# Down projections of a gated expert block: seven quarter-block products in place of eight half-block ones, and where the weights for them are prepared

## The chip, the cores and the metric

The kernel runs on one core of a Trainium2 chip (trn2). Its engines run side by side, each through its own list of instructions: TensorE (PE, with the weight loads shown apart as PEld), VectorE (DVE), ScalarE (ACT), GpSimd (POOL) and SyncE (SP), which here only issues transfers. They meet at semaphores. The metric is the device time of one launch in microseconds (us), lower is better; the time of the kernel before is the median of 3 runs.

## What is computed

Cut to what matters:

```
x = local attention with memory keys      # 3072 tokens x 512, kept on chip in Y
x = (x @ w_a * (x @ w_b)) @ w_out         # first block, hidden width 1536
P = exp(x @ w_gate - max); 8 Sinkhorn rounds over tokens and 8 experts
out = 0
for e in range(8):                        # second block
    h = maximum(x @ w1[e], 0)             # w1[e] is 512 x 1024
    out += P[:, e:e+1] * (h @ w2[e])      # w2[e] is 1024 x 512
```

Everything is float32. Products on TensorE are made of three passes over operands that are split into a high part, rounded to fp32r, and a low part that is the rest: high by high, high by low, low by high (`PARTS`).

## The kernel before

The 3072 tokens are three pairs of 1024 (two blocks of 512 each). The second block walks pair by pair, and in a pair through 32 units (`V2`): a unit is a quarter of an expert, 256 of its 1024 hidden columns. So there are 96 units (`M2`), numbered u = 0 to 95 here; pair 0 is u = 0 to 31. A unit has two halves of work on TensorE:

- The up projection, x by the w1 slice, as a 2x2 by 2x2 block product by Winograd's scheme with seven products (`PRODUCTS`, `product`, 6 matmuls of 512 columns each, 42 in all). ScalarE and VectorE join the products in PSUM (`seed`, `copy_u`, `copy_v`, `sum_22`, `sum_21`).
- The down projection, hidden by the w2 slice, as eight plain products (`down`, one for each 128 tokens, 6 matmuls of 512 columns, 48 in all). VectorE adds each to the output in SBUF, times the gate (`accumulate`). ScalarE makes the rectified hidden block's high parts (`h_hi`) and VectorE its low parts (`h_lo`).

On TensorE's list the two are woven together: up product 0 of unit u, down product 0 of unit u-1, up product 1, down product 1, and so on, then an eighth down product.

The weights need preparing once: in pair 0 (`fresh`) each slice is loaded raw from HBM, its operands for the seven products are made (sums on GpSimd in `up_sums`, high parts on ScalarE in `up_hi` and `down_hi`, low parts on GpSimd in `up_lo` and `down_lo`), and the finished form is also written to HBM (`w1_kept`, 1792 KB a unit; `w2_kept`, 1024 KB a unit). Pairs 1 and 2 only fetch it (`fetch_up`, `fetch_down`). The raw loads have two slots, one for w1 and one for w2 in the second block.

The order in pair 0 is written out by hand. On SP, for each u: load the raw w1 slice of u, keep w2 of u-1, load the raw w2 slice of u, keep w1 of u. All transfers sit in this one list, and a wait in it holds all that stand behind it. On GpSimd, for each u: `up_sums` of u+1, `down_lo` of u, `up_lo` of u+1. On ScalarE, for each u: `seed`, `down_hi` of u, first half of `up_hi` of u+1, `copy_u` (the fifth up product of u waits for it), second half of `up_hi`, then the hidden block's parts between `copy_v` and the end. TensorE's first product of unit u+1 waits for all of `up_lo` of u+1 (semaphore `w1_lo`).

Of the kernel before, what the change touches and what calls it, by code (L numbers as in the profile page):

```python
# [12 lines left out]
P = 128  # L13
# [26 lines left out]

def build(nc, q, k, v, mem_k, mem_v, w_a, w_b, w_out, w_gate, w1, w2, out):
    B, H, S, HD = q.shape
# [16 lines left out]
    HP = H // 2  # L59
# [23 lines left out]
    with ExitStack() as ctx:  # L83
# [49 lines left out]
        w2_kept = nc.dram_tensor("w2_kept", [V1 + V2, P, 4 * D], F32).ap()  # L135
# [3 lines left out]
        b_down = bank[3:6]  # L139
        b_lg, b_gate = bank[6], bank[7]  # L140
# [42 lines left out]

        x_sum = sem("x_sum")
# [18 lines left out]
        y_acc = sem("y_acc")  # L203
        s_wg = sem("s_wg")
# [59 lines left out]
        def kept_w2(w):  # L264
            return w % V1 if w < M1 else V1 + (w - M1) % V2
# [74 lines left out]
        def _(sp):  # L340
# [43 lines left out]
            def raw_free(item):  # L384
# [135 lines left out]
        def _(pool):  # L520
# [46 lines left out]
            def clear(r):  # L567
# [5 lines left out]
                else:  # L573
# [3 lines left out]
                                        pattern=[[0, H], [0, none.shape[2]]],  # L577
# [37 lines left out]
            for p in range(1, PAIRS):  # L615
                for i in range(len(X_POOL)):
                    operand_lo(3 + p, p, i)

        @block.tensor
        def _(pe):  # L620
# [145 lines left out]
            def down(w, g):  # L766
# [689 lines left out]
```

## Time and profile before

| | |
|---|---|
| median of 3 runs | 2724.42 us (2721.48 to 2724.61) |
| the profiled execution's own time | 2725.75 us |
| its span, first to last instruction | 2723.8 us |
| TensorE busy | 2660.6 us, 98% |
| TensorE granted clock, mean | 0.991 of full speed |
| VectorE, ScalarE, GpSimd busy | 51%, 28%, 19% |
| mean traffic to and from HBM | 161 GB/s |

The profile is of one execution. "Busy" of an engine is the union of its instructions' times. A matmul's time in the rows runs from its start to the arrival of its last result, so matmuls in a row overlap; what one of them costs is the distance between two starts. The granted clock 1.00 is the level of 2.4 GHz and 0.50 that of 1.2 GHz.

### The profile page before, as it was taken

How to read it: one execution, taken by the hardware profiler on the slowest of the kernel's cores; microseconds unless marked ns; L12 is line 12 of the kernel's file. 1: busy time of each engine (PE TensorE's matmuls, PEld its weight loads, DVE VectorE, ACT ScalarE, POOL GpSimd, SP SyncE). 2: the span in 40 equal slices, each digit the busy share in tenths (PEclk: the TensorE clock that was granted, in tenths of full speed). 3: DMA queues.
4: the chain of work that ended last, by engine and by line, in shares of the span. 5: the costliest groups of instructions: out<-in, count | busy, mean ns of one | idle time of the engine just before them, and what ended most of it. 6: DMA issues, size and time to landing. Idle time of an engine off the chain costs nothing.

```text
span 2723.8 us, 36964 instructions
## 1 busy us (share of the span) xinstructions
PE 2660.6 (98%) x15264; PEld 2194.9 (81%) x15264; DVE 1390.1 (51%) x2039; ACT 774.5 (28%) x1349; POOL 516.9 (19%) x440
## 2 busy tenths in 40 slices
PE   7879999999999999999999999999999999999999
PEld 6768878878777888888888888888888888888887
DVE  3454454544567545545565544544546445445444
ACT  4544432222333333333332222212223212212221
POOL 0055510110444454454430000000001000000000
PEclk9989999999999999999999999999999999999999
DMA  7655643443365555556544343343343443343342
GB/s 182 157 153 207 230 178 139 161 159 140 114 208 174 188 184 207 189 185 209 185 178 159 130 168 128 130 167 128 131 166 128 164 164 128 135 163 128 138 160 89
DMA packets 145542, 437.96 MB, mean 161 GB/s; under 512 B 53216, under 2 KB 101088, under 8 KB 113888
## 3 DMA queue, kind: packets, MB, share of 16 engines
q1 hardware_dynamic: 145376, 435.61, 44.5%
q8 instruction: 121, 1.98, 0.3%
q14 instruction: 45, 0.37, 0.0%
HBM read 308.69 MB, written 126.94 MB: 160 GB/s over the span
## 4 chain that ended last, share of the span: by engine, by line
PE 92%; DVE 4%; issue 1%; ACT 1%; DMA 1%; POOL 1%; SPq 1%; DVEq 0%; ACTq 0%
PE bank L719 44%; PE bank L794 44%; PE bank L642 2%; PE bank L681 1%; DVE tmp L1229 1%; PE bank L657 1%; PE bank L669 0%; DMA Qr<-in_q_dram 0%; DVE Y L1320 0%; DVE Y L1262 0%; PE bank L691 0%; SPq L371 0%; POOL X L563 0%; DVE hid L1325 0%; DVE hid L1381 0%
## 5 line engine op out<-in xcount | busy, mean ns | idle before, releaser
L719 PE MATMUL bank<-X,W 128*128 128x512 f32 x5550 | 1399.8, 391 | 14.7 <-ACT tmp L1032 4.8
L719 PEld LDWEIGHTS bank<-X,W 128*128 128x128 f32 x5550 | 1042.0, 188 | 241.0 <-issue 20.5
L794 PE MATMUL bank<-W,hid 128*128 128x512 f32 x4608 | 1154.2, 389 | 2.8 <-DVE Y L1259 2.8
L794 PEld LDWEIGHTS bank<-W,hid 128*128 128x128 f32 x4608 | 864.8, 188 | 182.9 <-DVE Y L1259 3.2
L1259 DVE SCALAR_TENSOR_TENSOR Y<-bank,gate,Y 128x512 f32<-128x512 f32 x720 | 539.4, 750 | 568.6 <-PE bank L794 561.0
L563 POOL TENSOR_TENSOR X<-Y,X 128x1024 fp32r<-128x1024 f32 x30 | 77.9, 2601 | 1022.6 <-ACT X L984 1022.6
L1090 ACT ACTIVATE hid<-tmp 128x512 fp32r<-128x512 f32 x192 | 121.3, 632 | 354.3 <-DVE tmp L1226 274.2
L794 PE MATMUL bank<-hid,W 128*128 128x512 f32 x864 | 219.3, 389 | 1.2 <-issue 1.2
L1028 ACT ACTIVATE tmp<-bank 128x512 f32<-128x512 f32 x132 | 79.0, 599 | 486.9 <-PE bank L719 486.9
L1381 DVE SCALAR_TENSOR_TENSOR hid<-bank,hid 128x512 fp32r<-128x512 f32 x192 | 132.7, 691 | 162.5 <-ACT hid L1090 162.4
L794 PEld LDWEIGHTS bank<-hid,W 128*128 128x128 f32 x864 | 162.4, 188 | 35.5 <-issue 1.6
L1090 ACT ACTIVATE hid<-bank 128x512 fp32r<-128x512 f32 x192 | 114.9, 598 | 230.6 <-PE bank L719 230.6
L1262 DVE TENSOR_TENSOR Y<-Y,bank 128x512 f32<-128x512 f32 x144 | 98.2, 684 | 153.9 <-PE bank L794 153.5
L1221 DVE TENSOR_TENSOR tmp<-bank,tmp 128x512 f32<-128x512 f32 x132 | 91.3, 692 | 165.3 <-ACT tmp L1032 165.1
L1017 ACT ACTIVATE bank<-bank 128x512 f32<-128x512 f32 x131 | 76.2, 582 | 316.5 <-PE bank L719 316.5
L1032 ACT ACTIVATE tmp<-bank 128x512 f32<-128x512 f32 x132 | 78.9, 597 | 261.4 <-PE bank L719 261.4
L1381 DVE SCALAR_TENSOR_TENSOR hid<-tmp,hid 128x512 fp32r<-128x512 f32 x192 | 145.5, 758 | 6.4 <-ACT hid L1090 0.7
L1226 DVE TENSOR_TENSOR tmp<-bank,tmp 128x512 f32<-128x512 f32 x132 | 91.2, 691 | 70.5 <-PE bank L719 69.6
L552 POOL TENSOR_TENSOR W<-Ws,W 128x512 fp32r<-128x512 f32 x88 | 114.3, 1322 | 23.3 <-ACT W L956 23.3
L557 POOL TENSOR_TENSOR W<-raw,W 128x1024 fp32r<-128x1024 f32 x38 | 91.3, 2402 | 68.0 <-ACT W L965 67.9
L552 POOL TENSOR_TENSOR W<-raw,W 128x512 fp32r<-128x512 f32 x88 | 88.7, 1030 | 42.8 <-ACT W L956 42.8
L541 POOL TENSOR_TENSOR Ws<-raw 128x256 f32<-128x256 f32 x44 | 33.9, 770 | 253.7 <-DMA raw<-in_moe_w_dram 251.7
(87 smaller groups left out, 1066.7 us busy)
## 6 DMA issues: line engine op xcount, KB each, us to landing
W<-w_kept SPq DMA_DIRECT2D x88, 1792.0 KB, 8.6
w_kept<-W SPq DMA_DIRECT2D x44, 1792.0 KB, 6.7
W<-w_kept SPq DMA_DIRECT2D x76, 1024.0 KB, 4.8
w_kept<-W SPq DMA_DIRECT2D x38, 1024.0 KB, 4.9
raw<-in_moe_w_dram SPq DMA_DIRECT2D x64, 512.0 KB, 6.4
Vw<-in_v_dram SPq DMA_DIRECT2D x176, 56.0 KB
Kr<-in_k_dram SPq DMA_DIRECT2D x12, 512.0 KB, 4.8
Qr<-in_q_dram SPq DMA_DIRECT2D x12, 512.0 KB, 4.5
```

Of the source, the lines that this page charges most:

```text
L552: nc.gpsimd.tensor_tensor(w_piece(c, n, 1), w_piece_of(slot, n), w_piece(c, n, 0).bitcast(F32), ALU.subtract).then_inc(w1_lo, 1)
L557: nc.gpsimd.tensor_tensor(W2[:, w % 2, 1, :], raw[:, item_w2(w) % 2, :], W2[:, w % 2, 0, :].bitcast(F32), ALU.subtract).then_inc(w2_lo, 1)
L719: last = nc.tensor.matmul(into[:, :], W1[:, c % 2, ws, w_slot, kc, :], X[:, pos, xs, kc, :], start=(start and kc == 0 and n == 0), stop=(k ...
L794: last = nc.tensor.matmul(into[:, :], lhsT, rhs, start=(j == 0 and n == 0), stop=(j == 1 and n == 2))
L1028: nc.scalar.activation(into, bank[BANK_B][:, :], ACT.Copy).then_inc(c_u, 1)
L1032: nc.scalar.activation(into, bank[BANK_B][:, :], ACT.Copy).then_inc(c_v, 1)
L1090: nc.scalar.activation(hid[:, u % 2, f, l, 0], of, ACT.Relu).then_inc(e_hi, 1)
L1221: nc.vector.tensor_tensor(into, bank[BANK_E][:, :], of, ALU.add).then_inc(c_22, 1)
L1226: nc.vector.tensor_tensor(into, bank[BANK_E][:, :], of, ALU.add).then_inc(c_21, 1)
L1259: nc.vector.scalar_tensor_tensor(out=y, in0=ps, scalar=by, in1=y, op0=ALU.mult, op1=ALU.add).then_inc(y_acc, 1)
L1262: nc.vector.tensor_tensor(y, y, ps, ALU.add).then_inc(y_acc, 1)
L1381: nc.vector.scalar_tensor_tensor(out=hid[:, u % 2, f, l, 1], in0=of, scalar=0.0, in1=hid[:, u % 2, f, l, 0].bitcast(F32), op0=ALU.max, op1 ...
```

## The change

Pair 0's down projections stay as they are. In pairs 1 and 2 (64 units) the down projection becomes a 2x2 by 2x2 block product with seven products as well: the hidden block is cut in halves of tokens and of hidden columns, w2's slice in halves of hidden columns and of output columns. Each of the seven (`down_product`, order and banks in `DOWN`) is 12 matmuls of 256 columns. The products are summed where they land, in PSUM, in two pairs of banks; ScalarE copies the shared first product from one pair to the other (`copy_halves`), and VectorE adds quarter blocks to the output straight from PSUM, 24 additions of 256 columns a unit (`add_blocks`). The seven left operands (`H`) are made in every unit: rectified blocks on ScalarE, four sums (`hidden_sum`) and seven low parts (`hidden_lo`) on GpSimd, seven high parts (`hidden_hi`) on ScalarE. VectorE's `h_lo` goes away there.

The right operands are made in pair 0, beside what was done: GpSimd makes four sums of w2's quarter blocks (`block_sums`) between `up_sums` and `down_lo`, ScalarE their high parts into the raw slot (`t_hi`, placed behind the sixth up product's hidden part), GpSimd their low parts (`block_sums_lo`) as the last step of the unit. Two more transfers a unit keep them (`keep_t_hi`, `keep_t_lo`, 512 KB each), and the raw w2 slot comes free only when both have been made and the first is kept. Pairs 1 and 2 fetch 1792 KB in place of 1024 KB for the down side (`fetch_blocks`). Buffers are laid out anew.

```diff
+DOWN = ((0, 0, 1), (1, 5, 1), (2, 3, 1), (4, 1, 0), (5, 2, 1), (6, 4, 0), (3, 6, 0))
...
+                    if item_w2(w) == item - 2 and w >= M1:
+                        sp.wait_ge(t_lo, w - M1 + 1)
+                        sp.wait_ge(s_th, 16 * (w - M1 + 1))
...
+            def keep_t_hi(u):
+                sp.wait_ge(t_hi, u + 1)
+                sp.dma_start(w2n_kept[u, :, 0, 4:8], b_blocks(M1 + u)).then_inc(s_th, 16)
+
+            def keep_t_lo(u):
+                sp.wait_ge(t_lo, u + 1)
+                sp.dma_start(w2n_kept[u, :, 1, 4:8], T_SUMS).then_inc(s_tl, 16)
...
             for u in range(1, V2):
                 load_up(C1 + u)
                 keep_down(M1 + u - 1)
+                keep_t_hi(u - 1)
                 load_down(M1 + u)
+                keep_t_lo(u - 1)
                 keep_up(C1 + u)
...
+            def block_sums(u):
...
+                nc.gpsimd.tensor_tensor(t1, b12, b11, ALU.subtract).then_inc(t_sum, 1)
+                nc.gpsimd.tensor_tensor(t3, b22, b12, ALU.subtract).then_inc(t_sum, 1)
+                pool.wait_ge(t_sum, 4 * u + 1)
+                nc.gpsimd.tensor_tensor(t2, b22, t1, ALU.subtract).then_inc(t_sum, 1)
+                pool.wait_ge(t_sum, 4 * u + 3)
+                nc.gpsimd.tensor_tensor(t4, b21, t2, ALU.subtract).then_inc(t_sum, 1)
+
+            def block_sums_lo(u):
+                pool.wait_ge(t_hi, u + 1)
+                nc.gpsimd.tensor_tensor(T_SUMS.bitcast(F32R), T_SUMS, b_blocks(M1 + u), ALU.subtract).then_inc(t_lo, 1)
...
             for u in range(V2):
                 if u + 1 < V2:
                     up_sums(C1 + u + 1)
+                block_sums(u)
                 down_lo(M1 + u)
                 if u + 1 < V2:
                     up_lo(C1 + u + 1)
...
+                block_sums_lo(u)
...
+            def down_product(u, q):
...
+                for half in range(2):
...
+                    ps = b_half[pair][half]
+                    for m in range(2):
+                        at = (2 * half + m) * P
+                        for n, (a, b) in enumerate(PARTS):
+                            last = nc.tensor.matmul(ps[:, m * D // 2:(m + 1) * D // 2], H[:, h, a, at:at + P],
+                                                    W2n[k % 2][:, b, blk, :],
+                                                    start=(q in (0, 5) and m == 0 and n == 0),
+                                                    stop=(m == 1 and n == 2), skip_group_check=True)
+                    last.then_inc(p_half, 1)
...
+                act.wait_ge(t_sum, 4 * u + 4)
+                act.wait_ge(w2_lo, kept_w2(w) + 1)
+                nc.scalar.activation(b_blocks(w).bitcast(F32R), T_SUMS, ACT.Copy).then_inc(t_hi, 1)
```

How the lists stand, at the places that the prediction speaks of. First SP's list in pair 0, one unit of it, before; `raw` with four by 256 is the w1 slice, with two by 512 the w2 slice, and `w_kept` is what is kept in HBM:

```order
L413 DMA w_kept<-W 128x3584 [waits w1_lo]
L403 DMA raw<-in_moe_w_dram 128x4x256 [waits w1_lo]
L418 DMA w_kept<-W 128x2048 [waits w2_lo]
L409 DMA raw<-in_moe_w_dram 128x2x512 [waits w2_lo]
L413 DMA w_kept<-W 128x3584 [waits w1_lo]
```

The same stretch of SP's list in the changed kernel, where `w2n_kept` takes the blocks for the seven products:

```order
L465 DMA w_kept<-W 128x3584 [waits w1_lo]
L455 DMA raw<-in_moe_w_dram 128x4x256 [waits w1_lo]
L474 DMA w2n_kept<-W_0 256x1x1024 [waits w2_lo]
L479 DMA w2n_kept<-raw 128x1024 [waits t_hi]
L461 DMA raw<-in_moe_w_dram 128x2x512 [waits s_th,t_lo,w2_lo]
L483 DMA w2n_kept<-tmp 128x1024 [waits t_lo]
L465 DMA w_kept<-W 128x3584 [waits w1_lo]
```

The raw load of w2, and with it all that stands behind it, now waits for `t_lo`; before, it waited for `w2_lo` alone.

GpSimd's list for one unit of pair 0 before (`Ws` holds w1's sums, `W` and `W2` are the split weights):

```order
L541 TENSOR_TENSOR Ws<-raw 128x256 [waits w1_lo,w1_hi,s_raw0]
L542 TENSOR_TENSOR Ws<-raw 128x256
L544 TENSOR_TENSOR Ws<-Ws,raw 128x256 [waits w_sum]
L546 TENSOR_TENSOR Ws<-raw,Ws 128x256 [waits w_sum]
L557 TENSOR_TENSOR W<-raw,W 128x1024 [waits w2_hi]
L552 TENSOR_TENSOR W<-raw,W 128x512 [waits w1_hi]
L552 TENSOR_TENSOR W<-raw,W 128x256 [waits w1_hi]
L552 TENSOR_TENSOR W<-Ws,W 128x512 [waits w1_hi] x2
```

And in the changed kernel, from behind `up_sums` (four rows as above, now lines 631 to 636) to the end of the unit:

```order
L664 TENSOR_TENSOR tmp<-raw 128x256 [waits s_tl,s_raw1]
L665 TENSOR_TENSOR tmp<-raw 128x256
L667 TENSOR_TENSOR tmp<-raw,tmp 128x256 [waits t_sum]
L669 TENSOR_TENSOR tmp<-raw,tmp 128x256 [waits t_sum]
L651 TENSOR_TENSOR W_1<-raw,W_1 128x1024 [waits w2_hi]
L642 TENSOR_TENSOR W<-raw,W 128x512 [waits w1_hi]
L642 TENSOR_TENSOR W<-raw,W 128x256 [waits w1_hi]
L642 TENSOR_TENSOR W<-Ws,W 128x512 [waits w1_hi] x2
L674 TENSOR_TENSOR tmp<-tmp,raw 128x1024 [waits t_hi]
```

Four instructions of 256 columns came in ahead of `down_lo`, and one of 1024 behind `up_lo`.

## Rows read from the trace of the kernel before

**Rows 1.** The page: busy times, and the chain that ended last by engine.
```profile
PE 2660.6 (98%) x15264; PEld 2194.9 (81%) x15264; DVE 1390.1 (51%) x2039; ACT 774.5 (28%) x1349; POOL 516.9 (19%) x440
...
PE 92%; DVE 4%; issue 1%; ACT 1%; DMA 1%; POOL 1%; SPq 1%; DVEq 0%; ACTq 0%
```

**Rows 2.** Windows in pair 0 and pair 2: engines' busy us, clock, DMA share, GB/s.
```profile
1200.00:1400.00 200.00, 200.00 (x883) 165.40 (x882) 103.32 (x140) 70.62 (x118) 96.10 (x81) 1.00 0.54 189
...
2200.00:2600.00 400.00, 400.00 (x1766) 331.21 (x1765) 196.05 (x274) 83.45 (x138) 0.00 (x0) 1.00 0.36 143
```

**Rows 3.** TensorE at 512 columns: timeline (start, us), and the down line's instructions.
```profile
1033.78 1.52 PE L719 MATMUL bank<-X,W 128*128 128x512 f32 x6
...
2704.04 13.76 PE L794 MATMUL bank<-W,hid 128*128 128x512 f32 x60
...
L794 PE MATMUL bank<-W,hid x4608: 387/389/628, 756.4 to 2717.4; 128*128 128x512 f32 x192
```

**Rows 4.** TensorE with full weight loads and short matmuls: timeline, and one line's durations.
```profile
5.93 1.39 PE L696 MATMUL bank<-ident 128*128 128x128 f32 x11
...
L696 PE MATMUL bank<-ident x32: 275/421/582, 1.6 to 7.1; 128*128 128x128 f32 x32
...
416.89 0.95 PE L816 MATMUL bank<-fold,lg 128*128 128x8 f32 x8
417.77 1.06 PE L806 MATMUL bank<-Y,wg 128*32 128x512 f32 x8
```

**Rows 5.** Timeline of POOL over one unit of pair 0.
```profile
1012.12 0.74 POOL L541 TENSOR_TENSOR Ws<-raw 128x256 f32<-128x256 f32 x1 [8.35 <-DMA raw<-in_moe_w_dram]
...
1014.78 0.74 POOL L546 TENSOR_TENSOR Ws<-raw,Ws 128x256 f32<-128x256 f32 x1
1016.57 2.40 POOL L557 TENSOR_TENSOR W<-raw,W 128x1024 fp32r<-128x1024 f32 x1 [1.05 <-ACT W L965]
1018.92 1.98 POOL L552 TENSOR_TENSOR W<-raw,W 128x512 fp32r<-128x512 f32 x2
1021.64 2.54 POOL L552 TENSOR_TENSOR W<-Ws,W 128x512 fp32r<-128x512 f32 x2 [0.74 <-ACT W L956]
1032.39 0.74 POOL L541 TENSOR_TENSOR Ws<-raw 128x256 f32<-128x256 f32 x1 [8.21 <-DMA raw<-in_moe_w_dram]
```

**Rows 6.** Timeline of SP's queue in the same unit, and DMA windows behind it.
```profile
1024.20 0.32 SPq L413 DMA_DIRECT2D w_kept<-W  x1
1024.57 0.43 SPq L403 DMA_DIRECT2D raw<-in_moe_w_dram  x1
...
1025.00:1026.00 1.00, 1.00 (x6) 0.84 (x5) 0.22 (x1) 0.18 (x1) 0.00 (x0) 1.00 1.15 459
...
1030.00:1031.00 1.00, 1.00 (x6) 0.84 (x5) 0.65 (x1) 0.00 (x0) 0.00 (x0) 1.00 0.81 280
```

**Rows 7.** Timeline of POOL at the start of pair 0.
```profile
748.64 3.00 POOL L552 TENSOR_TENSOR W<-Ws,W 128x512 fp32r<-128x512 f32 x2
...
768.61 2.54 POOL L552 TENSOR_TENSOR W<-Ws,W 128x512 fp32r<-128x512 f32 x2
```

**Rows 8.** ScalarE: `copy_u` and the first half of `up_hi` in the timeline.
```profile
1020.44 0.60 ACT L1028 ACTIVATE tmp<-bank 128x512 f32<-128x512 f32 x1 [3.13 <-PE bank L719]
...
1036.79 0.93 ACT L956 ACTIVATE W<-raw 128x512 fp32r<-128x512 f32 x2
```

**Rows 9.** VectorE's group that reads 256 columns of PSUM, by form.
```profile
L1168 DVE TENSOR_TENSOR On<-bank,rsum 128x256 f32<-128x256 f32 x48 | 18.1, 419 | 21.0 <-PE bank L681 20.5
```

**Rows 10.** Windows around an idle stretch of TensorE early in the kernel.
```profile
68.00:69.00 1.00, 0.00 (x0) 0.00 (x0) 0.00 (x0) 1.00 (x4) 0.89 (x1) 1.00 1.11 184
...
72.00:74.00 2.00, 2.00 (x61) 1.67 (x60) 0.72 (x3) 1.38 (x5) 0.52 (x1) 0.53 1.17 217
```

**Rows 11.** DMA: the fetch of 1792 KB, from issue to landing; the timeline's stores.
```profile
W<-w_kept SPq DMA_DIRECT2D x88, 1792.0 KB, 8.6
...
2714.54 6.48 SPq L439 DMA_DIRECT2D out_dram<-Y  x8
```

More of the change, by code:

```diff
@@ L139, in build @@
         b_down = bank[3:6]
+        b_half = bank[3:5], bank[5:7]
         b_lg, b_gate = bank[6], bank[7]
@@ L182, in build @@
         s_w2l = [sem(f"s_w2l{i}") for i in range(2)]
+        t_sum = sem("t_sum")
+        t_hi = sem("t_hi")
+        t_lo = sem("t_lo")
+        s_th = sem("s_th")
+        s_tl = sem("s_tl")
+        s_w2n = [sem(f"s_w2n{i}") for i in range(2)]
         x_sum = sem("x_sum")
@@ L884, in _ @@
                         total(TOTALS.index((u, pos)))
-                down(w - 1, NG - 1)
-            for g in range(NG):
-                down(M1 + M2 - 1, g)
+                if u <= V2:
+                    down(w - 1, NG - 1)
+            for q in range(NP):
+                down_product(M2 - 1, q)
         @block.scalar
@@ L1110, in _ @@
                     act.wait_ge(e_lo, 4 * (u - 1))
-                copy_u(c, tmp[:, u_at])
+                copy_u(c, u_at)
                 if u + 1 < V2:
@@ new lines, in copy_halves @@
+            def copy_halves(k):
+                for half in range(2):
+                    act.wait_ge(p_half, 2 * NP * k + half + 1)
+                    if k > 0:
+                        act.wait_ge(z_acc, 24 * (k - 1) + 22 + 2 * half)
+                    nc.scalar.activation(b_half[0][half][:, :], b_half[1][half][:, :], ACT.Copy).then_inc(c_ba, 1)
+            for u in range(V2, M2):
+                w, c, k = M1 + u, C1 + u, u - V2
+                n, p = first_use(w + 1), u // V2 + 1
+                a12, a22 = U_AT[k % 2], VN_AT[k % 2]
+                seed(c)
+                if k > 0:
+                    copy_halves(k - 1)
+                operands_late(w)
+                if n is not None:
+                    operand_hi(n, p, 0, c)
+                if k > 0:
+                    hidden_hi(k - 1, 5)
+                if k < 2:
+                    act.wait_ge(e_lo, 4 * V2 + 4 * k - 4)
+                else:
+                    act.wait_ge(h_lo, NP * (k - 2) + H_LO.index(5) + 1)
+                copy_u(c, a12)
+                if n is not None:
+                    operand_hi(n, p, 1, c)
+                act.wait_ge(p_prod, NP * c + 4)
+                if k == 0:
+                    act.wait_ge(e_lo, 4 * V2)
+                else:
+                    act.wait_ge(h_sum, 4 * k - 1)
+                    act.wait_ge(h_lo, NP * (k - 1) + 1)
+                nc.scalar.activation(A11, bank[BANK_A][:, :], ACT.Relu).then_inc(r_rl, 1)
+                hidden_hi(k, 0)
+                if k > 1:
+                    act.wait_ge(h_lo, NP * (k - 1))
+                copy_v(c, a22)
+                if n is not None:
+                    operand_hi(n, p, 3, c)
+                act.wait_ge(c_22, c + 1)
+                nc.scalar.activation(a22, a22, ACT.Relu).then_inc(r_rl, 1)
+                act.wait_ge(p_prod, NP * c + 6)
+                if k == 0:
+                    act.wait_ge(s_tl, 16 * V2)
+                else:
+                    act.wait_ge(h_lo, NP * (k - 1) + H_LO.index(6) + 1)
+                nc.scalar.activation(A21, bank[BANK_B][:, :], ACT.Relu).then_inc(r_rl, 1)
+                if n is not None:
+                    operand_hi(n, p, 2, c)
+                hidden_hi(k, 2)
+                hidden_hi(k, 1)
+                act.wait_ge(c_21, c + 1)
+                nc.scalar.activation(a12, a12, ACT.Relu).then_inc(r_rl, 1)
+                hidden_hi(k, 4)
+                hidden_hi(k, 6)
+                hidden_hi(k, 3)
+                if n is not None:
+                    operand_hi(n, p, 4, c)
```

323 lines of the change are left out of this document (262 added, 61 removed).

## The prediction

> **What bounds the kernel now.** I began with the page: TensorE is busy 98% of the span and 92% of the chain that ended last [rows 1]. Then I cut the span into windows. From 1200 us on TensorE has no idle time, and a window of 400 us holds 1766 matmuls [rows 2], so one costs 226.5 ns. The timeline agrees: 60 down matmuls of 512 columns take 13.76 us, and with the 0.389 us of the last one taken off, 59 distances make 226.6 ns each [rows 3]. A unit of the second block is 42 + 48 = 90 such matmuls, or 20.39 us.
>
> TensorE is the bound everywhere in that block, but the windows show a difference between pairs: in pair 0 GpSimd is busy 96 of 200 us, in pair 2 not at all [rows 2]. Pair 0 prepares the weights, so I read its timeline for the way from one slice to the next. GpSimd ends the low parts of a w1 slice at 1021.64 + 2.54 = 1024.18. At once SP keeps that slice (1.8 MB) and loads the next raw one [rows 6]; GpSimd's first sum on it starts at 1032.39, after 8.21 us idle that ended with the DMA [rows 5]. Then come the sums (1012.12 to 15.52 a unit earlier, 3.4 us), `down_lo` 2.4, `up_lo` 2.0 + 2.5. Together 8.2 + 3.4 + 2.4 + 4.5 = 18.5 us without any wait for ScalarE. That is a loop of its own, and it is shorter than the 20.39 us of TensorE by just 1.9 us. It is hidden now, and barely: the last low part of one slice at 748.64 + 3.00 = 751.64 and of the next at 768.61 + 2.54 = 771.15 are 19.5 us apart, at the beginning of pair 0 [rows 7].
>
> **What the change gives on TensorE.** In 64 units, 48 matmuls of 512 columns become 84 of 256. Columns fall to 7/8, weight loads rise by 75%. The old ones cost 48 x 0.2265 = 10.87 us. For the new no row exists, so I bound one matmul from the neighbours. Above: if all that a 512-column matmul costs over its 213.3 ns of columns (13.2 ns) is fixed, 106.7 + 13.2 = 119.9 ns. Below: what full weight loads allow. Eight matmuls of 8 columns with full loads start 416.89 and their follower 417.77, 110 ns each; the warm-up matmuls run at (1.39 - 0.275) / 10 = 111.5 ns [rows 4]. That last is the nearest row: one of them lasts 275 ns at the least, and less the 176 ns that a 512-column matmul lasts beyond its 213 of columns (389 in all [rows 3]) that leaves a stream of about 99 ns, close to the 106.7 of 256 columns, behind as large a load. It costs 4.8 ns over 106.7. Between 4.8 at its 128 columns and 13.2 at 512 a straight line gives 7.4 at 256: **114.1 ns**. So 84 x 0.1141 = 9.58 us, a gain of 1.29 us a unit and **-82.6 us** over 64 (-100 at 111.5 ns, -51 at 119.9). It turns into a loss above 10.87 / 84 = 129.4 ns.
>
> A rule speaks against this. The Trainium skill (TensorE: Matmul & The Clock Gate, Part 3) says that a weight load overlaps matmuls in flight only when its row group differs; here all loads fill the array. By it a 256-column matmul would wait out its load. The trace contradicts it at 512 columns, since 213 + 110 = 323 ns would be needed where 226.5 stand; I keep it as a rival with a small chance.
>
> The other engines in pairs 1 and 2, with a unit of 42 x 0.2265 + 9.58 = 19.1 us: ScalarE has 16 instructions of about 0.6 us [rows 8], 9.8 us. VectorE has 24 additions of 256 columns at 0.42 or a little more [rows 9] and two sums, 11.5 to 13 us. GpSimd has 11 of 512 columns, at 1.27 us by the pair of 2.54 [rows 5], 14 us, and they can't begin before the sixth up product. All fit, but the chain is tight: sixth up product at about 15.0 us of the unit, rectified 15.7, three GpSimd sums to 19.5, low part 1 at 20.8, wanted by TensorE at 23.2. The first product's copy between banks is ready at about 3.4 us of the next unit and wanted at 4.1. Margins 2.4 and 0.7 us; I charge nothing in the steady state. At the edges I charge 9 us: 4 at the start of pair 1, where `fetch_blocks` waits for the last `keep_t_lo` (some 12 us into unit 32) and `fetch_up` for unit 33 stands behind it (one such fetch takes 8.6 us [rows 11], the second some 4 more at 459 GB/s [rows 6], so it lands at 24 to 25 against 20.4 wanted); 2 at the change of pairs, where GpSimd also has five pieces of 2.4 to 2.6 us; 3 in the last unit, whose seven products have no up products between them to hide the copies and low parts. The additions and stores behind the end (6 us now [rows 3, 11]) stay.
>
> **What it costs in pair 0.** TensorE's list is unchanged there, 20.39 us a unit. But the hidden loop grows. On SP's list the raw w1 load of u+1 stands behind `load_down` of u, which now waits for `t_lo` of u-1. On GpSimd `t_lo` is made behind `up_lo` of u. So the raw load no longer starts when `up_lo` of u ends, but one instruction later, and with more in front of it. Step by step, from one `up_lo` end to the next:
>
> - `block_sums_lo`, 1024 columns, as `down_lo`: 2.4 us [rows 5].
> - Transfers until the first sum can start. Before: 8.2 us with 1.8 + 0.5 MB. Now the raw w2 load and `keep_t_lo`, 0.5 MB each, go ahead: 1.1 us at 459 GB/s for the write, 1.9 at 280 for the load [rows 6], so 11.2 us. Low end 8.2 (hidden in the queue), high end 13 (all 3.3 MB at 280 GB/s and a start).
> - `up_sums` 3.4, `block_sums` (four of 256 columns at 0.74 and gaps, as `up_sums`) 3.3, `down_lo` 2.4, `up_lo` 4.5: 13.6 us [rows 5].
>
> Sum 27.2 us, 24.2 to 29.0, against 20.39. Since each step waits for the one before and GpSimd is busy for 16 us of it, nothing overlaps. **Pair 0 goes at the pace of the weights, not of TensorE.** `t_hi` on ScalarE doesn't lengthen it: it waits for `w2_lo`, which is done 4.5 us before `up_lo` ends. ScalarE is held up as well: the first half of `up_hi` stands ahead of `copy_u` and waits for the raw load, which lands 13.6 us before the next unit starts, 13.6 us into this one; `copy_u` ends 0.93 + 0.60 us later [rows 8], at 15.1, and the fifth up product wanted it at 10.9. TensorE then waits 4.2 us in mid-unit and some 2.6 at its end. Early in the kernel an idle stretch of about 2 us was followed by a clock of 0.53 for some 3 us [rows 10]; a unit can lose 1.7 us of matmuls to that and still end inside 27.2.
>
> How many units: the weights of unit 1 are ready at 751.6 + 3.3 = 754.9, just when unit 1 starts now (756.4 less one product, 755.0 [rows 3]). `t_lo` of 0 is at 757.3, the first sum for unit 2 at 768.5, its `up_lo` done at 782.1. From unit 2 to 31 are 29 steps: 782.1 + 29 x 27.2 = 1570.9. Now unit 14 starts at 1033.78 [rows 3] and unit 31 at 1033.8 + 17 x 20.39 = 1380.4. So **+190.5 us** (+103 at 24.2, +243 at 29.0). Unit 31 prepares no w1 slice and runs at its old pace.
>
> **Sum.** Against the profiled execution's 2725.75 (1.3 over the median, nothing at this size): 2725.75 + 190.5 - 82.6 + 9 = **2842.7 us**, so 2843, 4% slower.
>
> **Rivals.**
> - The preparation stays hidden, and the gain comes through: 2725.75 - 82.6 + 9 = 2652 us. It is one mechanism, a pair-0 loop no longer than 20.4 us; up to 20.4 + 73.6 / 29 = 22.9 us the kernel is not slower. For it: GpSimd is idle half of pair 0 [rows 2], and idle engines look like room. Against: the idle time is the wait for the raw load, and the load is now issued behind the added work. The transfers and GpSimd's 16 us would have to overlap, and the lists don't let them. Chance 0.09, with what lies between it and 22.9 us.
> - A 256-column matmul does not hide its weight load: 106.7 + 110 = 217 ns, 84 x 0.217 = 18.2 us, +7.4 us a unit in place of -1.3, so 2843 + 64 x 8.7 = 3400 us. Rows at 512 columns speak against it. 0.04.
> - It hides it only in part, with 130 to 140 ns (the loads of the 8-column group plus a stall): 84 x 0.135 = 11.3 us, 2843 + 64 x 1.76 = 2956 us. The warm-up row speaks against it. 0.04.
> - The chain through GpSimd and ScalarE in pairs 1 and 2 misses its slot, by 1 us a unit or so, if GpSimd's instructions of 512 columns take over 1.7 us beside a busier VectorE: about 2905 us. Margins of 0.7 and 2.4 us are for it. 0.10; it lies in the range.
>
> **How the numbers follow.** The forecast (loop 24 to 29 us, matmul 111 to 120 ns) has 0.73. Its own range is 2743 (24.2 and 111.5 ns) to 2935 (29.0, 119.9 ns, 8 more at edges). 2745 to 2930 takes in the late-chain rival too and leaves out the hidden one and the dear matmuls. A measurement of this kernel tells 0.2% from no change. Slower holds the forecast, the late chain and both dear matmuls, less a little for mixed cases: 0.90. Faster 0.09, same 0.01.
>
> **What the changed profile would show.** Right: from 770 to 1570 us units of about 27 us, TensorE at 75% busy there and waiting for `w1_lo` at the unit's start and for `copy_u` in its middle; `up_sums` waiting for the raw load 11 us behind `t_lo`; behind it TensorE at 99% and units of 19.1 us, 12 down matmuls in 1.37 us. Wrong: pair 0 still at 20.4 us; raw loads that land while GpSimd still works on the slice before; a down matmul over 120 ns; waits for GpSimd's `H` parts or ScalarE's bank copies in pairs 1 and 2. The step that I trust least in size is the 11.2 us of transfers: each us of it is 29 us of the total.

## The result and the profile after

The changed kernel takes 2910.53 us (median of 4 runs, 2904.53 to 2911.09) against 2724.14 us for the kernel before (4 runs as well, one more than stood above). The ratio is 1.068, 95% interval 1.066 to 1.070: **6.8% slower**. The prediction said slower, 2843 us, with a range of 2745 to 2930 that holds the result near its upper end. The profiled execution took 2910.31 us.

The page's first line and its chain by engine stand here against [rows 1]. In the chain GpSimd and the DMAs now hold 30%, where they held 2%.

```profile
PE 2694.1 (93%) x17568; PEld 2300.3 (79%) x17568; DVE 1480.3 (51%) x2807; ACT 1123.9 (39%) x1957; POOL 1582.1 (54%) x1304
...
PE 62%; POOL 19%; DMA 11%; DVE 3%; SPq 2%; issue 2%; ACT 1%; POOLq 0%; DVEq 0%; ACTq 0%
```

Windows in pair 0 and in pair 2, in the columns of [rows 2]. In pair 0 TensorE is now idle 61 to 70 of 400 us, so busy 85% and 83%, and its mean clock is below 1.00; in pair 2, from 2500 to 2880 us, it is never idle.

```profile
800.00:1200.00 400.00, 339.12 (x1356) 269.74 (x1355) 190.63 (x277) 118.51 (x191) 229.96 (x205) 0.93 0.48 185
1200.00:1600.00 400.00, 330.07 (x1299) 262.18 (x1298) 160.28 (x208) 120.72 (x192) 231.00 (x204) 0.90 0.48 181
...
2500.00:2880.00 380.00, 380.00 (x2429) 345.41 (x2428) 216.32 (x501) 176.09 (x306) 269.29 (x214) 1.00 0.51 188
```

The loop in pair 0, from the timeline of GpSimd; it answers to [rows 5]. L631 is the first of `up_sums`, L664 of `block_sums`, L651 is `down_lo`, L642 `up_lo`, L674 `block_sums_lo`.

```profile
1012.95 0.73 POOL L631 TENSOR_TENSOR Ws<-raw 128x256 f32<-128x256 f32 x1 [11.05 <-DMA raw<-in_moe_w_dram]
...
1015.81 0.73 POOL L664 TENSOR_TENSOR tmp<-raw 128x256 f32<-128x256 f32 x1
...
1018.69 2.40 POOL L651 TENSOR_TENSOR W<-raw,W 128x1024 fp32r<-128x1024 f32 x1
1021.06 2.44 POOL L642 TENSOR_TENSOR W<-raw,W 128x512 fp32r<-128x512 f32 x2
1023.46 2.54 POOL L642 TENSOR_TENSOR W<-Ws,W 128x512 fp32r<-128x512 f32 x2
1025.95 2.84 POOL L674 TENSOR_TENSOR tmp<-tmp,raw 128x1024 fp32r<-128x1024 f32 x1
1039.97 0.72 POOL L631 TENSOR_TENSOR Ws<-raw 128x256 f32<-128x256 f32 x1 [11.18 <-DMA raw<-in_moe_w_dram]
```

From one first sum to the next, 1012.95 to 1039.97, are 27.0 us: 15.8 of work without a gap and 11.2 of waiting for the raw load. SP's queue in the same unit shows why it waits. All four transfers are issued in one go, the first (raw w2, L461) at 1028.86, just behind `block_sums_lo`'s end at 1028.79, and the raw w1 load (L455) is the last.

```profile
1028.86 0.38 SPq L461 DMA_DIRECT2D raw<-in_moe_w_dram  x1
1029.29 0.47 SPq L483 DMA_DIRECT2D w2n_kept<-tmp  x1
1029.81 0.43 SPq L465 DMA_DIRECT2D w_kept<-W  x1
1030.28 1.18 SPq L455 DMA_DIRECT2D raw<-in_moe_w_dram  x1
```

TensorE in that unit: a wait of 4 us in mid-unit that ends with `copy_u` (L1231), then seven more pieces of six matmuls, then a short wait for `up_lo` (L642) at the unit's start. The piece behind the long wait takes 2.78 us and the next one 2.02, where six such matmuls take 1.52 elsewhere; together they cost 1.7 us. The granted clock was 0.50 or 0.51 from 1015 to 1018 us, the level of 1.2 GHz, and 1.00 from 1018 us on (the last two rows are windows, in the columns of [rows 2]).

```profile
1014.38 2.78 PE L885 MATMUL bank<-X,W 128*128 128x512 f32 x6 [4.04 <-ACT tmp L1231]
1016.95 2.02 PE L962 MATMUL bank<-W,hid 128*128 128x512 f32 x6
...
1026.05 1.65 PE L885 MATMUL bank<-X,W 128*128 128x512 f32 x6 [0.27 <-POOL W L642]
...
1041.40 2.55 PE L885 MATMUL bank<-X,W 128*128 128x512 f32 x6 [4.18 <-ACT tmp L1231]
...
1016.00:1017.00 1.00, 1.00 (x4) 0.71 (x4) 0.00 (x0) 1.00 (x3) 1.00 (x2) 0.50 0.00 0
1018.00:1019.00 1.00, 1.00 (x6) 0.83 (x5) 1.00 (x3) 0.00 (x1) 1.00 (x2) 1.00 0.00 0
```

The last `up_lo` instructions of unit 2 and of unit 31:

```profile
779.51 2.53 POOL L642 TENSOR_TENSOR W<-Ws,W 128x512 fp32r<-128x512 f32 x2
...
1568.92 2.54 POOL L642 TENSOR_TENSOR W<-Ws,W 128x512 fp32r<-128x512 f32 x2
```

Their ends, 782.04 and 1571.46, are 29 units apart: **27.2 us a unit** over all of pair 0, against 20.4 before.

In pairs 1 and 2 the timeline of TensorE is even, but for their edges. A piece of the seven-product part takes 1.44 us (2001.45 to 2002.89) and an up product 1.38 (2002.89 to 2004.27), so a unit is 7 x 2.82 = **19.74 us**.

```profile
2001.45 1.60 PE L988 MATMUL bank<-W2n,H 128*128 128x256 f32 x12
2002.89 1.55 PE L885 MATMUL bank<-X,W 128*128 128x512 f32 x6
2004.27 1.60 PE L988 MATMUL bank<-W2n,H 128*128 128x256 f32 x12
```

Two edges cost more than I had charged. Where pair 1 starts, TensorE waited three times (units 31, 32 and 33), once for ScalarE's `copy_v` (L1235) and twice for a fetch of w1; each wait was followed by a slow piece.

```profile
1592.18 2.93 PE L885 MATMUL bank<-X,W 128*128 128x512 f32 x6 [6.74 <-ACT tmp L1235]
...
1605.64 2.93 PE L885 MATMUL bank<-X,W 128*128 128x512 f32 x6 [3.53 <-DMA W<-w_kept]
...
1631.82 2.49 PE L885 MATMUL bank<-X,W 128*128 128x512 f32 x6 [4.12 <-DMA W<-w_kept]
```

Where pair 2's operand (x in the form that its up products read) is built, in unit 63, three timelines are read together. GpSimd came to the operand's first low part (L679) only behind the hidden block's last three (L759). VectorE's first sum of the operand (L1468) waited for it 10.45 us, with the block additions queued behind it, and TensorE waited for those.

```profile
2231.17 3.76 POOL L759 TENSOR_TENSOR H<-tmp,H 128x512 fp32r<-128x512 f32 x3
2234.86 2.36 POOL L679 TENSOR_TENSOR X<-Y,X 128x1024 fp32r<-128x1024 f32 x1
...
2237.26 1.23 DVE L1468 TENSOR_TENSOR Y<-Y 128x1024 f32<-128x1024 f32 x1 [10.45 <-POOL X L679]
...
2239.41 2.90 PE L988 MATMUL bank<-W2n,H 128*128 128x256 f32 x12 [6.56 <-DVE Y L1573]
```

### The profile page after: what moved, and what is told of

It reads as the page before. It is cut to its first block, busy times and chain, and to the rows that moved or that the text cites. A ratio compares the mean times of both kernels' runs of the same rounds, so it can differ in the third digit from the quotient of the medians.

```text
span 2908.6 us, 44866 instructions
## 1 busy us (share of the span) xinstructions
PE 2694.1 (93%) x17568; PEld 2300.3 (79%) x17568; DVE 1480.3 (51%) x2807; ACT 1123.9 (39%) x1957; POOL 1582.1 (54%) x1304
## 4 chain that ended last, share of the span: by engine, by line
PE 62%; POOL 19%; DMA 11%; DVE 3%; SPq 2%; issue 2%; ACT 1%; POOLq 0%; DVEq 0%; ACTq 0%
PE bank L885 32%; PE bank L988 21%; DMA raw<-in_moe_w_dram 10%; PE bank L962 6%; POOL W L642 5%; POOL tmp L674 3%; POOL W L651 3%; PE bank L808 2%; POOL Ws L631 1%; POOL tmp L669 1%; POOL Ws L636 1%; POOL tmp L667 1%; POOL X L679 1%; POOL tmp L665 1%; POOL tmp L664 1%
## 5 line engine op out<-in xcount | busy, mean ns | idle before, releaser
L1573 DVE SCALAR_TENSOR_TENSOR Y<-bank,gate,Y 128x256 f32<-128x256 f32 x1504 | 623.4, 477 | 411.4 <-PE bank L988 410.0
L988 PEld LDWEIGHTS bank<-W2n,H 128*128 128x128 f32 x5376 | 705.5, 192 | 50.2 <-issue 11.5
L988 PE MATMUL bank<-W2n,H 128*128 128x256 f32 x5376 | 717.2, 283 | 11.9 <-DVE Y L1573 10.5
L759 POOL TENSOR_TENSOR H<-tmp,H 128x512 fp32r<-128x512 f32 x352 | 449.5, 1299 | 143.4 <-ACT H L1357 143.4
L962 PE MATMUL bank<-W,hid 128*128 128x512 f32 x1536 | 411.7, 409 | 0.0
L962 PEld LDWEIGHTS bank<-W,hid 128*128 128x128 f32 x1536 | 309.3, 202 | 69.5
L1357 ACT ACTIVATE H<-tmp 128x512 fp32r<-128x512 f32 x352 | 211.9, 628 | 218.9 <-POOL tmp L754 125.4
L679 POOL TENSOR_TENSOR X<-Y,X 128x1024 fp32r<-128x1024 f32 x30 | 78.0, 2606 | 388.2 <-ACT X L1185 388.2
L1546 DVE SCALAR_TENSOR_TENSOR Y<-bank,gate,Y 128x512 f32<-128x512 f32 x224 | 167.2, 747 | 184.6 <-PE bank L962 184.0
L631 POOL TENSOR_TENSOR Ws<-raw 128x256 f32<-128x256 f32 x44 | 34.3, 780 | 344.2 <-DMA raw<-in_moe_w_dram 342.2
L1231 ACT ACTIVATE tmp<-bank 128x512 f32<-128x512 f32 x132 | 78.3, 593 | 154.6 <-PE bank L885 154.6
L642 POOL TENSOR_TENSOR W<-raw,W 128x512 fp32r<-128x512 f32 x88 | 103.1, 1192 | 45.2 <-ACT W L1156 45.2
L759 POOL TENSOR_TENSOR H<-ex,H 128x512 fp32r<-128x512 f32 x96 | 126.0, 1312 | 0.0
L1513 DVE TENSOR_TENSOR tmp<-bank,tmp 128x512 f32<-128x512 f32 x132 | 91.2, 691 | 54.6 <-PE bank L885 53.4
L642 POOL TENSOR_TENSOR W<-Ws,W 128x512 fp32r<-128x512 f32 x88 | 113.5, 1311 | 0.0
```

The source lines that it names most:

```text
L642: nc.gpsimd.tensor_tensor(w_piece(c, n, 1), w_piece_of(slot, n), w_piece(c, n, 0).bitcast(F32), ALU.subtract).then_inc(w1_lo, 1)
L679: nc.gpsimd.tensor_tensor(X[:, pos, 1], x_source(p, pos), X[:, pos, 0].bitcast(F32), ALU.subtract).then_inc(x_lo, 1)
L759: nc.gpsimd.tensor_tensor(H[:, pos, 1], of, H[:, pos, 0].bitcast(F32), ALU.subtract).then_inc(h_lo, 1)
L962: last = nc.tensor.matmul(into[:, :], lhsT, rhs, start=(j == 0 and n == 0), stop=(j == 1 and n == 2))
L988: last = nc.tensor.matmul(ps[:, m * D // 2:(m + 1) * D // 2], H[:, h, a, at:at + P], W2n[k % 2][:, b, blk, :], start=(q in (0, 5) and m == ...
L1357: nc.scalar.activation(H[:, pos, 0], of, ACT.Copy).then_inc(h_hi, 1)
```

## The experiments

The theory: pair 0 is paced by a loop over `t_lo`, SP's queue and GpSimd's list. The rivals: the added work is too much for its engines wherever the load stands; ScalarE's late `copy_u` is the cost, as the list of waits names it; the loss lies in the seven-product part.

**e1_load_ahead.** One transfer moved in SP's list.

```diff
+            load_up(C1 + 1)
             for u in range(1, V2):
-                load_up(C1 + u)
                 keep_down(M1 + u - 1)
+                if u + 1 < V2:
+                    load_up(C1 + u + 1)
                 keep_t_hi(u - 1)
                 load_down(M1 + u)
                 keep_t_lo(u - 1)
                 keep_up(C1 + u)
```

> One line of SP's list moved in pair 0: the raw w1 load of unit u+1 stands ahead of keep_t_hi, so it waits for up_lo of unit u alone, not for t_lo behind it; the same work and the same bytes. Theory (the loop over t_lo and SP's queue sets pair 0's pace): the loop breaks, GpSimd's 16.4 us a unit fit under TensorE's 20.4 us, pair 0 goes back from 27.2 to 20.4-20.6 us a unit, 29 units, so 2910 - 191 and some 10 less at the start of pair 1, where the late raw w2 load held ScalarE: about 2710 us (2700 to 2730), faster than the kernel before. Rival (the added work itself on GpSimd and ScalarE is too much for a unit, wherever the load stands): pair 0 stays over 24 us a unit, the whole over 2810 us.

Measured: 2729.18 us (2716.92 to 2745.48, 10 runs), ratio to before 1.002 (0.9997 to 1.005); the profiled execution 2719.67. Pair 0 is back at TensorE's pace: in the window from 1200 to 1350 us TensorE has no idle time, and two successive `block_sums` in the timeline of GpSimd start 20.2 us apart, with 3 us idle in front of each.

```profile
1200.00:1350.00 150.00, 150.00 (x663) 124.23 (x662) 78.42 (x103) 59.28 (x95) 112.43 (x105) 1.00 0.65 247
...
1165.69 0.74 POOL L666 TENSOR_TENSOR tmp<-raw 128x256 f32<-128x256 f32 x1 [3.22 <-DMA w2n_kept<-tmp]
...
1185.90 0.74 POOL L666 TENSOR_TENSOR tmp<-raw 128x256 f32<-128x256 f32 x1 [3.04 <-DMA w2n_kept<-tmp]
```

All the work and all the bytes are as in the changed kernel, and 181 us of the 186 are gone. So the loss was not the added work but where one load stood in the list. The runs spread over 28 us, more than any other kernel's here.

**e2_load_before_keeps.** The load stays behind the wait for `t_lo`, but goes ahead of `keep_t_lo` and `keep_up`, 2.3 MB together.

```diff
+            load_up(C1 + 1)
             for u in range(1, V2):
-                load_up(C1 + u)
                 keep_down(M1 + u - 1)
                 keep_t_hi(u - 1)
                 load_down(M1 + u)
+                if u + 1 < V2:
+                    load_up(C1 + u + 1)
                 keep_t_lo(u - 1)
                 keep_up(C1 + u)
```

> The raw w1 load of unit u+1 still stands behind load_down and so behind the wait for t_lo, but ahead of keep_t_lo and keep_up (2.3 MB). Theory (the 11.2 us are bytes in the queue ahead of the load): the load lands about 5.5 us behind t_lo in place of 11.2, the loop is 16.4 + 5.5 = 21 to 22 us a unit, the whole 2910 - 29 x 5.5 = 2750 us (2735 to 2775). Rival (the wait for t_lo itself costs most, bytes little): pair 0 at 25 us a unit or more, over 2845 us.

Measured: 2760.18 us (2756.60 to 2764.37), ratio 1.014 (1.012 to 1.016). GpSimd's timeline shows the first sum 6.3 to 6.8 us behind `t_lo` in place of 11.2, and units of 22.2 us (1006.51 to 1028.67):

```profile
1006.51 0.74 POOL L633 TENSOR_TENSOR Ws<-raw 128x256 f32<-128x256 f32 x1 [6.80 <-DMA raw<-in_moe_w_dram]
...
1028.67 0.75 POOL L633 TENSOR_TENSOR Ws<-raw 128x256 f32<-128x256 f32 x1 [6.26 <-DMA raw<-in_moe_w_dram]
```

So 5.0 us of the loop's 27.2 were bytes ahead in the queue; over 29 units that is 145 of the 150 us gained. The wait for `t_lo` with one short transfer keeps the loop 1.8 us over TensorE's 20.4. TensorE's waits here are named after `up_lo`, 31.7 us.

**e3_up_hi_behind_copy_v.** ScalarE's list alone.

```diff
                 down_hi(w)
-                if u + 1 < V2:
-                    up_hi(c + 1, (0, 1))
...
                 copy_u(c, u_at)
-                if u + 1 < V2:
-                    up_hi(c + 1, (2, 3))
...
                 copy_v(c, v_at)
+                if u + 1 < V2:
+                    up_hi(c + 1)
```

> ScalarE's list only: all four up_hi pieces of u+1 behind copy_v of u, so copy_u no longer waits for the raw w1 load. The profile puts 100 us of TensorE's waits in pair 0 down to copy_u. Theory (the loop over GpSimd and SP sets the pace, and TensorE only waits in another place): the wait of about 4 us in mid-unit moves to the unit's start, behind up_lo; units stay at 27.2 us and the whole within 10 us of 2910. Rival (copy_u's late start is the cost): about 100 us faster, 2810 us.

Measured: 2906.00 us (2904.42 to 2908.13), ratio 1.067 (1.065 to 1.069): no change that matters. The list of TensorE's waits from 755 us on (us in total, times, the longest), first of the changed kernel:

```profile
PE bank L885 <- ACT tmp L1231: 114.2, 28, 5.4
```

and of this one:

```profile
PE bank L885 <- POOL W L642: 121.6, 28, 6.2
```

The 114 us that the list put down to `copy_u` on ScalarE (100 of them from 780 to 1500 us) went to another name and stayed; 0.6 us are left under the old one. That rival falls.

**e4_preparation_alone.** The kernel before, with pair 0's side of the change alone. GpSimd's list is shown; `t_hi`, the two keeps and the later release of the raw slot come with it as under "The change".

```diff
...
+                block_sums(u)
                 down_lo(M1 + u)
                 if u + 1 < V2:
                     up_lo(C1 + u + 1)
+                else:
+                    for i in range(len(X_POOL)):
+                        operand_lo(4, 1, i)
+                block_sums_lo(u)
```

> The kernel before with pair 0's added preparation alone (block_sums, t_hi, block_sums_lo, both keeps, raw w2 slot freed by them); pairs 1 and 2 keep the eight-product down projections and nothing reads the sums that are kept. Theory: pair 0 loses the 191 us as in the changed kernel, plus some 10 where pair 1 starts: about 2925 us (2910 to 2940); the difference to the changed kernel, which gains 41 us by cheaper units and loses some 20 at two edges, is then about 15 us. Rival (the loss lies in the seven-product part): near 2725 us.

Measured: 2934.86 us (2933.21 to 2940.25), ratio 1.078 (1.076 to 1.080). The preparation alone costs 211 us, more than the whole change, so the seven-product part of the changed kernel gives 24 us back, edges included. GpSimd waits 11.3 and 11.4 us for the raw load here, and its units are 27.3 us (1012.56 to 1039.88). The rival that seeks the loss in the seven-product part falls.

**e5_edges.** e1 with three lists put in another order. The diff shows SP's at the start of pair 1, then the first lines of VectorE's and GpSimd's at the change of pairs. Not shown: in unit 31 GpSimd makes the first low part of pair 1's operand ahead of `block_sums`, and two more of VectorE's steps change places.

```diff
+            fetch_up(C1 + V2)
             keep_down(M1 + V2 - 1)
             keep_t_hi(V2 - 1)
-            fetch_up(C1 + V2)
+            fetch_up(C1 + V2 + 1)
             keep_t_lo(V2 - 1)
...
+                add_blocks(u - 1, 1)
                 if n is not None:
                     operand_sum(n, p, 1)
-                add_blocks(u - 1, 1)
...
                 hidden_sum(k, 3)
+                if first_use(w + 2) is not None:
+                    operand_lo(first_use(w + 2), 2, 0)
                 hidden_lo(k, 6)
```

> e1_load_ahead with the edges mended, no work added or left out. At the start of pair 1 the fetches of w1 for units 32 and 33 are issued ahead of the keeps that held them, and GpSimd makes the first low part of pair 1's operand ahead of block_sums. At the change to pair 2 GpSimd makes the first low part of the operand in unit 62, ahead of the hidden block's last three, and VectorE puts the operand's sums and low part behind the block additions that TensorE waits for. Theory (the edges cost what the waits name: 3.4 + 4.5 + 4.1 us at the start of pair 1 and 6.6 + 2.8 us at the change of pairs in e1's profile, plus 3 to 5 us of lower clock behind them): 15 to 25 us off e1's profiled 2719.7, so about 2700 us (2693 to 2708). Rival (the operand's chain through VectorE only moves its wait): under 8 us off.

Measured: 2697.37 us (2693.83 to 2718.24, 6 runs), ratio to before **0.992 (0.990 to 0.995)**: faster than both kernels, the one before by 0.8% and the changed one by 7.3%. The profiled execution took 2696.92, 23 us under e1's. The first seven-product matmul starts at 1426.2 us in place of 1443.2 and from there to the last one are 1264.4 us in place of 1270.2. At the change of pairs TensorE's longest wait for VectorE went from 6.6 to 3.6 us. Not all of the 17 us before it needs to be the edge: e1's own executions differ by more.

**e6_width_probe.** Eight groups of 24 matmuls behind the end of the kernel before, such as

```python
            for i in range(24):
                nc.tensor.matmul(pa[:, 0:256], pw, px[:, 0:256], start=True, stop=True)
```

> The kernel before with eight groups of 24 matmuls behind its last one, each on the same operands: 512, 384, 320, 256, 192 and 128 columns under a full 128x128 load, then 256 and 128 columns under a load of 64 columns. Their results are not used. Theory A (a fixed 13.3 ns on each matmul over columns / 2.4 ns): distances 226.6, 173, 147, 120, 93 or the load's 110, 110 ns, and with half the load 256 columns still 120. Theory B (the 120 ns of 256 columns come from the weight load, not from the stream): 256 columns at half the load clearly under 120, near 110, and 192 columns under a full load not under 120.

Measured (one run, 2742.78 us with the probe's 26 us in it), from the timeline of TensorE:

```profile
2714.89 5.60 PE L891 MATMUL bank<-X,W 128*128 128x512 f32 x24
2720.33 4.35 PE L893 MATMUL bank<-X,W 128*128 128x384 f32 x24
2724.51 3.67 PE L895 MATMUL bank<-X,W 128*128 128x320 f32 x24
2728.03 3.04 PE L897 MATMUL bank<-X,W 128*128 128x256 f32 x24
2730.90 2.82 PE L899 MATMUL bank<-X,W 128*128 128x192 f32 x24
2733.56 2.81 PE L901 MATMUL bank<-X,W 128*128 128x128 f32 x24
2736.21 2.90 PE L903 MATMUL bank<-X,W 128*64 128x256 f32 x24
2738.95 1.60 PE L905 MATMUL bank<-X,W 128*64 128x128 f32 x24
```

The distance of two groups' starts over 24 gives 226.7 ns at 512 columns, 174.2 at 384, 146.7 at 320, 119.6 at 256, 110.8 at 192 and 110.4 at 128. From 512 to 256 that is columns / 2.4 ns plus 12.9 to 14.2 ns, whatever the width; below, 110.5 ns is a floor. With a load of 64 columns, 256 columns take 114.2 ns: the surcharge falls from 12.9 to 7.5. Neither theory holds whole. A is right for full loads, but with half the load 256 columns fell to 114.2 and did not stay at 120: 5.4 ns of the surcharge go with the width of the load, and what the other 7.5 are is not shown. B's test failed, for 192 columns were at the floor, under 120, and 256 were above it; so a 256-column matmul pays for its columns and 13 ns more, and is not held by the floor.

**e7_t_hi_early.** e5 with ScalarE's `t_hi` moved from behind the sixth product's hidden part to behind the first one's.

```diff
                 first_h_hi(u, 0, bank[BANK_A][:, :], 0, 0)
+                act.wait_ge(t_sum, 4 * u + 4)
+                act.wait_ge(w2_lo, kept_w2(w) + 1)
+                nc.scalar.activation(b_blocks(w).bitcast(F32R), T_SUMS, ACT.Copy).then_inc(t_hi, 1)
...
                 first_h_hi(u, 2, bank[BANK_B][:, :], 0, 1)
-
-                act.wait_ge(t_sum, 4 * u + 4)
-                act.wait_ge(w2_lo, kept_w2(w) + 1)
-                nc.scalar.activation(b_blocks(w).bitcast(F32R), T_SUMS, ACT.Copy).then_inc(t_hi, 1)
```

> e5_edges with ScalarE's t_hi moved ahead of copy_v, so that t_lo follows up_lo on GpSimd at once and the raw w2 load need not wait for keep_t_hi. In e1's profile the load is issued 4.4 us behind the end of t_hi's predecessor on GpSimd; now about 2.7 us earlier. Theory (pair 0 of e1 runs with TensorE as the bound but with so little slack that slower transfers push some runs by 20 us): the median comes down to that of the fastest runs and the spread of the runs shrinks, median 2695 to 2703 us. Rival (the spread is not pair 0's): same spread as e5, median within 4 us of e5's.

Measured: 2712.15 us (2704.77 to 2716.22, 6 runs), ratio to before 0.996 (0.994 to 0.997), so 15 us over e5's median, though the two intervals just meet. The forecast failed: the median did not come down. SP's queue shows that `keep_t_hi` (L479) went out behind the raw w1 load (L455), though `t_hi` had ended at 1159.1:

```profile
1162.40 0.39 SPq L455 DMA_DIRECT2D raw<-in_moe_w_dram  x1
1162.83 0.50 SPq L479 DMA_DIRECT2D w2n_kept<-raw  x1
1167.89 0.38 SPq L461 DMA_DIRECT2D raw<-in_moe_w_dram  x1
```

The raw w2 load (L461), which waits for that keep to land, still left 2.7 us behind the end of `t_lo`. And the unit grew: TensorE started 868 matmuls from 1200 to 1400 us, where e5 has 884.

**e8_keep_t_hi_first.** e7 with that one line turned.

```diff
+                keep_t_hi(u - 1)
                 if u + 1 < V2:
                     load_up(C1 + u + 1)
-                keep_t_hi(u - 1)
```

> e7_t_hi_early with one line of SP's list moved: keep_t_hi stands ahead of the raw w1 load again. In e7's profile keep_t_hi was issued 0.4 us behind that load, which waits for up_lo, 3.8 us after t_hi had ended, so the early t_hi freed nothing, and the raw w2 load still went out 2.7 us behind t_lo; ScalarE's wait for down_lo ahead of copy_v meanwhile stretched the unit to 20.8 us. Theory: keep_t_hi now lands while up_lo still runs, the raw w2 load goes out at t_lo's end, GpSimd reaches down_lo 2 to 3 us sooner, copy_v is no longer late and the unit is 20.4 us again: median 2693 to 2700 us, at or a little under e5's 2697, with a smaller spread. Rival (t_hi ahead of copy_v is itself the loss): stays near e7's 2712 us.

Measured: 2703.23 us (2701.03 to 2707.51, 5 runs), ratio 0.993 (0.992 to 0.995). GpSimd's wait ahead of `block_sums` fell from 3.2 to 3.8 us to 0.5 and 0.9, and TensorE is back at 884 matmuls from 1200 to 1400 us, so in mid-pair the mechanism is as said; the spread shrank to 6 us. The median missed its range by 3 us. In this profile the first seven-product matmul starts at 1436.1 us, 10 us later than in e5's, and the traces say where these lie: ahead of pair 0's body. The down line's first matmuls (L967) in e5, then in e8:

```profile
L967 PE MATMUL bank<-W,hid x1536: 387/389/793, 753.7 to 1423.8; 128*128 128x512 f32 x192
L967 PE MATMUL bank<-hid,W x864: 387/389/628, 202.5 to 752.1; 128*128 128x512 f32 x173
...
L967 PE MATMUL bank<-W,hid x1536: 387/389/796, 764.3 to 1433.6; 128*128 128x512 f32 x192
L967 PE MATMUL bank<-hid,W x864: 387/389/629, 207.8 to 762.8; 128*128 128x512 f32 x173
```

Of the 10.6 us between 753.7 and 764.3, 5.3 stand before the first block's down products already (202.5 and 207.8), in code that no edit touched; from 753.7 and 764.3 on, pair 0 takes as long in both. The other 5 come with `t_hi`'s new place. In the first unit it stands ahead of `copy_v` (L1240) and waits for `down_lo`, and TensorE waits 7.62 us for `copy_v`, where it waited 3.03 in e5; e7's profile has 7.63. The rows are ScalarE's in e8 and TensorE's in e8 and in e5:

```profile
751.93 1.06 ACT L1323 ACTIVATE raw<-tmp 128x1024 fp32r<-128x1024 f32 x1 [3.58 <-POOL W L654]
...
753.62 2.90 PE L890 MATMUL bank<-X,W 128*128 128x512 f32 x6 [7.62 <-ACT tmp L1240]
...
743.78 2.39 PE L890 MATMUL bank<-X,W 128*128 128x512 f32 x6 [3.03 <-ACT tmp L1240]
```

So the early `t_hi` costs about 5 us once, in the first unit. Leaving it in its old place there alone was not tried. e5 has the better median, e8 the narrower runs; the two don't differ beyond their intervals.

## Why the prediction was right, and by how much it was short

- **The bound and the mechanism.** Right. Pair 0 went at the pace of the weights. Predicted 27.2 us a unit, measured 27.2 over 29 units; start of unit 31 predicted 1570.9, measured 1571.5. The transfers, the step that I trusted least, took 11.1 and 11.2 us, with 11.2 forecast. The shares of the writes and the load within them were an estimate, and only e2 tests them: 2.3 MB ahead of the load came to 4.4 to 5.0 us. The smaller steps were off both ways and cancelled: `block_sums_lo` 2.8 for 2.4, `up_sums` and `block_sums` 2.9 each for 3.4 and 3.3, `up_lo` 4.9 for 4.5. The change of e1 shows the loop itself, and e2 the part that is bytes.
- **Where TensorE waits.** Right: 4.0 to 4.2 us for `copy_u` in mid-unit (4.2 predicted). At the unit's start it waited 0.3 us, not 2.6. The low clock behind the long wait took up 1.7 us of the difference, as much as the prediction had said that a unit could lose to it. So TensorE was busy 83 to 85% of pair 0, and not the 75% named as a sign: slow matmuls count as busy.
- **The matmul of 256 columns.** The term that was mis-sized. I took 114.1 ns, on a line between 4.8 ns over the stream at 128 columns and 13.2 at 512; the probe has 119.6, just under the upper bound of my range (119.9). The step that failed is the reading of the warm-up row: its 111.5 ns are the floor that a full load sets (110.4 in the probe), not a stream with 4.8 ns of surcharge, so it said nothing of what lies over a stream. A unit became 19.74 us, not 19.1, and over 63 units that is 40 us. The price at 256 columns makes 29 of them: with the probe's 119.6 and 226.7 ns a unit would be 19.57 us. The other 11 are a term that I had put at nothing: an up product beside the new pieces takes 1.38 us and not six times 226.6 ns, 1.36. Why is not shown. The gain on TensorE was 20.39 - 19.74 = 0.65 us a unit, 42 us over 64, less than the 51 that I had as the least. Two slips in the working are small beside it: the line gives 7.6 ns at 256 columns, not 7.4, and the gain at 111.5 ns is 96 us, not 100.
- **The rule about row groups** (the Trainium skill, TensorE: Matmul & The Clock Gate, Part 3), by which a weight load overlaps matmuls in flight only when its row group differs, is not borne out for these loads: with full loads 256 columns take 119.6 ns, not the sum of 107 and 110.
- **The edges.** Charged 9 us. At the start of pair 1 I charged 4 and it took 21: 19.5 in units 31 and 32 (60.3 us where two old units take 40.8) and 1.7 in unit 33, behind the last of the three waits (1631.82 to 1653.21, 21.4 us). I had seen the fetch of unit 33, but not the second fetch, and not the wait in unit 31: the last raw w2 load comes late, `block_sums` waits 5.6 us for `keep_t_lo` to land, and GpSimd makes the first low part of pair 1's operand only behind them. At the change of pairs I charged 2 and it took 14 (from 1631.8 to the last unit's start at 2890.9 are 1259.1 us, 63 x 19.74 are 1243.6, and 1.7 of the 15.5 between them are unit 33's): I had counted GpSimd's time there, but not that VectorE's list holds the block additions behind the operand's first sum. The last unit was as charged, 13.4 us for 9.6 + 3.
- **The sum.** 0.6 for pair 0, 40 for the units, 17 and 12 for the edges, -1 at the end (the last unit 0.8 longer, what stands behind it 1.7 shorter) make 69 of the 68 us between 2842.7 and 2910.3. All misses lay on one side. That the number stayed in the range is in part luck: with the loop at its measured 27.2 us, the dearest matmul and the 8 us more at the edges that the range had allowed, the sum comes to 2882; what carried the range to 2930 was the loop's high end, which did not come about.
- **The chain through GpSimd and ScalarE in pairs 1 and 2** kept its slots, as charged: TensorE has no idle time from 2500 to 2880 us. The rival of the late chain falls with it. That VectorE's 256-column addition takes 477 ns where I had 420 or a little more did no harm.
- **The hidden rival** (2652 us) was wrong for this kernel, but e1 shows how close its mechanism lay, one transfer's place in SP's list apart. Its time is another matter: e1 took 2729, since the matmuls and edges cost what they cost.

## What to carry to other kernels

Added work on an idle engine is free only if the next load isn't issued behind it: follow each transfer's issue point round the whole loop, and sum the loop, before counting busy shares. The engine that the list of waits names is where the wait shows, not where it comes from; here 114 us moved from ScalarE to GpSimd for a gain of under 5 us. A matmul's price at a new width was here the larger of two terms, its columns plus 13 to 14 ns, and a floor of 110 ns that a full load sets; a row at the floor says nothing of the first term. And an instruction moved up a list can hold what now stands behind it: the first unit, where its input comes late, has to be looked at by itself.

## What the runs showed of the hardware

Distances of fp32r matmuls with a full 128x128 load: 226.7, 174.2, 146.7 and 119.6 ns at 512, 384, 320 and 256 columns, then a floor of 110.4 to 110.8 ns. With 64 weight columns 256 columns take 114.2 ns, and 128 columns (1.60 - 0.222) / 23 = 59.9, with 222 ns for one of them. The Trainium skill (TensorE: Matmul & The Clock Gate, LDWEIGHTS) gives a load as its columns over 1.2 ns: an estimate of 107 and 53 ns from that page, 4 and 7 ns under the probe's 110.4 and 59.9. The first is a floor, for it stays from 192 to 128 columns; whether the second is one, no row tells, since 128 columns at 2.4 GHz are 53 ns as well. In pair 0 an idle stretch of 4.0 us was followed by three us at a clock of 0.50 (the us before them 0.79, the us behind 1.00), so that twelve matmuls took 4.4 us from start to start in place of 2.7.
